# A dense layer between two routed stages: q, x and y reach their transposed form through memory and VectorE instead of TensorE

## The reference, cut to what matters

```python
# q, k, v: (8, 8, 576, 64); x: 4608 tokens x 512; w_in: 512 x 2048; w_out: 2048 x 512
kv = einsum('bhsd,bhse->bhde', k, v)
o = einsum('bhsd,bhde->bhse', q, kv)
o = o / sqrt(mean(o * o, axis=-1) + 1e-6) * g_norm
x = o.transpose(0, 2, 1, 3).reshape(4608, 512)
h = x @ w_in
y = (maximum(h, 0) + alpha * minimum(h, 0)) @ w_out          # dense layer
e = argmax(y @ w_gate); p = softmax(y @ w_gate)[e]; s = sigmoid((y @ w_output_gate)[e])
out = p * s * (maximum(y @ w1[e], 0) @ w2[e])                # routed layer, 8 experts, F = 1024
```

## Time and profile before

| | |
|---|---|
| median of 3 runs | 1503.25 us (1499.38 to 1505.24) |
| the profiled execution's own time | 1500.92 us |
| its span | 1499.1 us |
| granted TensorE clock, mean | 0.994 of full speed |
| TensorE busy with matmuls | 1468.6 us, 98% |
| VectorE, ScalarE, GpSimd busy | 48%, 33%, 9% |
| dense tiles | from 30.3 us to about 966 us |
| a dense tile in the middle (tile 5's start to tile 6's) | 427.1 to 506.5 us |
| DMA | 104.5 MB, 100,516 packets |

### The profile page before, as it was taken

The page is one execution under the profiler, slowest core; times in us unless marked ns, Lnnn a source line. Parts: engine busy times, 40 slices in busy tenths (PEclk is TensorE's granted clock), DMA queues, the critical chain, the costliest instruction groups (busy, mean ns, idle before and its releaser), DMA issues.

```text
span 1499.1 us, 27268 instructions
## 1 busy us (share of the span) xinstructions
PE 1468.6 (98%) x8553; PEld 1277.5 (85%) x8554; DVE 723.5 (48%) x1796; ACT 491.3 (33%) x994; POOL 127.6 (9%) x143
## 2 busy tenths in 40 slices
PE   7899999999999999999999999999999999999997
PEld 6788989888898989898989898887888888888886
DVE  3585555565656465645555655663122114444411
ACT  3442232323232323223222221433233234444422
POOL 1000000000000000000000000112111111111111
PEclk8999999999999999999999999999999999999999
DMA  8532121102121102213100000524123114444410
GB/s 193 136 95 70 33 75 33 43 2 75 33 75 33 43 2 61 46 36 71 31 13 23 1 22 1 146 88 156 44 91 106 43 37 149 155 142 157 152 41 32
DMA packets 100516, 104.51 MB, mean 70 GB/s; under 512 B 55296, under 2 KB 75920, under 8 KB 100434
## 3 DMA queue, kind: packets, MB, share of 16 engines
q1 hardware_dynamic: 91618, 80.99, 19.6%
q0 software_dynamic: 7872, 21.09, 4.4%
q10 hardware_dynamic: 944, 1.33, 0.4%
HBM read 84.04 MB, written 20.65 MB: 70 GB/s over the span
## 4 chain that ended last, share of the span: by engine, by line
PE 90%; DMA 4%; DVE 2%; ACT 1%; issue 1%; SPq 1%; POOL 0%; ACTq 0%; POOLq 0%; DVEq 0%
PE psAcc L1346 25%; PE psH L1334 24%; PE psAcc L1469 15%; PE psH L1448 14%; PE psO L1458 2%; PE psO L1279 2%; PE psO L1249 1%; PE psQ L1429 1%; PE psQ L1265 1%; DMA AR<-rows,uid 1%; PE psY L1297 1%; DMA lists<-meta,slot 1%; PE psY L1289 1%; PE psY L1306 1%; DMA AR<-in_v_dram 1%
## 5 line engine op out<-in xcount | busy, mean ns | idle before, releaser
L1346 PE MATMUL psAcc<-W,XG 128*128 128x512 f32 x1728 | 438.9, 399 | 0.0
L1334 PE MATMUL psH<-XG,W 128*128 128x384 f32 x2304 | 436.3, 337 | 2.2 <-DVE W L958 1.4
L1334 PEld LDWEIGHTS psH<-XG,W 128*128 128x128 f32 x2304 | 408.4, 188 | 18.0 <-issue 2.7
L1346 PEld LDWEIGHTS psAcc<-W,XG 128*128 128x128 f32 x1728 | 313.7, 188 | 66.1 <-issue 6.0
L683 ACT ACTIVATE XG<-AR 128x128 fp32r<-128x128 f32 (+1 forms) x384 | 132.1, 364 | 639.9 <-DVE AR L988 634.2
L985 DVE TENSOR_SCALAR AR<-psH,acol 128x384 f32<-128x384 f32 x192 | 118.4, 617 | 296.0 <-PE psH L1334 296.0
L1448 PE MATMUL psH<-W,XG 128*128 (+1 forms) x996 | 250.4, 400 | 0.0
L1469 PE MATMUL psAcc<-W,XG 128*128 (+1 forms) x984 | 243.4, 396 | 0.0
L1469 PEld LDWEIGHTS psAcc<-W,XG 128*128 128x128 f32 x984 | 182.9, 189 | 37.3
L1448 PEld LDWEIGHTS psH<-W,XG 128*128 128x128 f32 x996 | 180.8, 188 | 36.8 <-DVE W L966 0.4
L1153 DVE TENSOR_TENSOR XG<-psO,XG 128x512 fp32r<-128x512 f32 x82 | 56.6, 690 | 222.1 <-ACT XG L742 218.8
(11 more groups left out here) (200 smaller groups left out, 873.3 us busy)
## 6 DMA issues: line engine op xcount, KB each, us to landing
AR<-in_moe_w_dram SPq DMA_DIRECT2D x68, 512.0 KB, 4.9
AR<-in_k_dram SPq DMA_DIRECT2D x16, 576.0 KB, 5.4
rows<-AR SPq DMA_DIRECT2D x36, 256.0 KB, 2.1
AR<-in_q_dram SPq DMA_DIRECT2D x32, 256.0 KB, 3.1
AR<-in_v_dram SPq DMA_DIRECT2D x14, 576.0 KB, 6.8
AR<-in_moe_w_in_dram SPq DMA_DIRECT2D x16, 256.0 KB, 2.9
AR<-in_moe_w_out_dram SPq DMA_DIRECT2D x16, 256.0 KB, 3.5
AR<-in_v_dram ACTq DMA_DIRECT2D x2, 576.0 KB, 9.3
```

The source lines that it names most:

```text
L1334: mm = pe.matmul(psH[f % 2][:, 0:TILE], w_in_v[:, wp, cc, f * P:(f + 1) * P], xT[:, b, xp, cc, :], start=(cc == 0 and (wp, xp) == PARTS[0] ...
L1346: mm = pe.matmul(psAcc[m][:, :], gT[:, f % 2, gp, m * P:(m + 1) * P], w_out_v[:, wp, f, :], start=(f == 0 and (gp, wp) == PARTS[0]), stop= ...
```

## The change

Tiles 1 to 11 no longer use PE transposes for q, x and y (the first tile's q and x, and the last tile's y, keep theirs). A 32x32 transpose on VectorE turns only squares within a quarter of the partitions, so the data is brought into memory order that makes this enough. q is loaded as blocks: partition quarter `quad` holds model dimensions 128 quad to 128 quad + 127, in runs of 32 floats (128 bytes), by 16 DMAs a tile, or 32 where the tile spans two batches; `q_turn` transposes each group into `qT`. Scaled x goes out to a scratch tensor `xr` in three DMAs and comes back in twelve (`turn_x`, `fetch_x`), `x_turn` writes it to `sq_sb`, and `x_evacuate` and `x_low` are two instructions each because the norm's weight now depends on the parity of the block (`gcol` has two columns). y, already stored to `rows`, comes back in twelve DMAs (`fetch_y`) and `y_turn` fills `yT`. The model dimension is thereby permuted over partitions, so `w_in` (four DMAs in place of one per chunk) and the gate weights (`wgq`) are loaded in the same order. `load_kv`'s first half moves ahead of `load_q`; `normalise`, `scale_rows`, `parts_copy`, `logit_parts` and `logits` move by a step or so; `wide_logits` moves from step 14 of tile 0 to step 0 of tile 1.

The diff, cut to its core:

```diff
+            def load_q(i, c):
+                a = 3 * i + c
+                if a == 1:
+                    sp.wait_ge(q_tr, TG)
+                else:
+                    sp.wait_ge(qT_set, TG * (a - 1))
+                for bl, s0, t0, n in q_place(c):
+                    src = q[2 * i + bl, :, s0:s0 + 32 * n, :].rearrange("(c r) (t i) (k n) -> r k i c t n", r=2, i=32, k=2)
+                    for quad in range(4):
+                        for cc in range(CH):
+                            sp.dma_start(q_blocks[32 * quad:32 * quad + 32, cc, t0:t0 + n, :],
+                                         src[quad // 2, quad % 2, :, cc, :, :]).then_inc(q_blocks_in, 16)
+            def turn_x(a):
+                for j in range(TG):
+                    sp.wait_ge(xn_set, 3 * a + j + 1)
+                    sp.dma_start(xr[j * P:(j + 1) * P, :], o_sb[:, j, :]).then_inc(x_saved, 16)
+            def fetch_x(a):
+                sp.wait_ge(x_saved, 16 * TG * a)
+                for j in range(TG):
+                    for quad in range(4):
+                        sp.dma_start(o_sb[32 * quad:32 * quad + 32, j, :].rearrange("p (t n) -> p t n", t=4),
+                                     by_quadrant(xr[j * P:(j + 1) * P, :])[quad]).then_inc(x_back[j], 16)
+            def fetch_y(t):
+                sp.wait_ge(y_saved, 16 * TG * (t + 1))
+                for m in range(TG):
+                    src = by_quadrant(rows[TILE * t + P * m:TILE * t + P * (m + 1), 0:DM])
+                    for quad in range(4):
+                        sp.dma_start(y_sb[32 * quad:32 * quad + 32, m, :].rearrange("p (t n) -> p t n", t=4),
+                                     src[quad]).then_inc(y_back[m], 16)
...
-                sp.dma_start(st[:, 0:DM].rearrange("p (c n) -> p c n", c=CH),
-                             w_in[:, f * P:(f + 1) * P].rearrange("(c p) n -> p c n", p=P)
-                             ).then_inc(stage_in[f % 2], 16)
+                for quad in range(4):
+                    sp.dma_start(st[32 * quad:32 * quad + 32, 0:DM].rearrange("p (c n) -> p c n", c=CH),
+                                 w_in[P * quad:P * quad + P, f * P:(f + 1) * P].rearrange("(c i) n -> i c n", c=CH)
+                                 ).then_inc(stage_in[f % 2], 16)
...
             for f in range(5, FC):
                 load_dense(f)
+                if f == FC - 2:
+                    turn_x(1)
...
                 if before:
                     store_y(t - 1)
+                    fetch_y(t - 1)
+                else:
+                    fetch_x(1)
+                if kv:
+                    load_kv(4 * i + 2 * c + 2, 2 * i + c + 1, 0)
                 if ahead and (kv or c == 0):
                     load_q(*nxt(*nxt(i, c)))
                 if kv:
-                    for half in range(2):
-                        load_kv(4 * i + 2 * c + 2 + half, 2 * i + c + 1, half)
+                    load_kv(4 * i + 2 * c + 3, 2 * i + c + 1, 1)
+                if before and ahead:
+                    turn_x(t + 1)
+                    fetch_x(t + 1)
...
# ScalarE, x_evacuate: two halves from sq_sb, where one read psY
-                act.wait_ge(x_tr, 3 * a + j + 1)
+                    act.wait_ge(x_turned, 3 * (a - 1) + j + 1)
+                for k in range(2):
+                    ins = nc.scalar.activation(by_parity(xT[:, b, 0, :, j * P:(j + 1) * P])[:, k, :, :], src[:, k, :, :],
+                                               ACT.Copy, scale=gcol[:, k:k + 1])
...
+            def q_turn(i, c, j):
+                a = 3 * i + c
+                dve.wait_ge(q_blocks_in, q_count(i, c))
+                dve.wait_ge(o_mm, 3 * a + j)
+                V.transpose(out=qT.rearrange("p c (t i) -> p c t i", i=32), in_=q_blocks[:, :, 4 * j:4 * j + 4, :]
+                            ).then_inc(qT_set, 1)
+            def x_turn(a, j):
+                dve.wait_ge(x_back[j], 64 * a)
+                dve.wait_ge(x_lo, 3 * a + j)
+                V.transpose(out=sq_sb.rearrange("p (c t i) -> p c t i", c=CH, i=32), in_=turned(o_sb[:, j, :])
+                            ).then_inc(x_turned, 1)
+            def y_turn(t, m):
+                dve.wait_ge(y_back[m], 64 * (t + 1))
+                dve.wait_ge(lg_parts, 3 * t + m)
+                V.transpose(out=yT.rearrange("p c (t i) -> p c t i", i=32), in_=turned(y_sb[:, m, :])).then_inc(yT_set, 1)
...
# VectorE, the order in a tile
                     step(i, c, f)
+                    if ahead and g in (0, 1, 2):
+                        q_turn(*nxt(i, c), g)
                     if ahead and g in (1, 2, 3):
                         squares(a, g - 1)
-                    if before and f in (1, 3, 5):
-                        yT_copy(t - 1, (f - 1) // 2)
-                    if before and f in (2, 4, 6):
-                        parts_copy(t - 1, (f - 2) // 2)
+                    if t == 1 and f == 0:
+                        wide_logits()
+                    if before and f in (4, 5, 6):
+                        parts_copy(t - 1, f - 4)
+                    if before and f in (3, 4, 5):
+                        y_turn(t - 1, f - 3)
...
                     if ahead and f in (13, 14, 15):
+                        x_turn(a, f - 13)
                         x_low(a, (i + c + 1) % 2, f - 13)
...
# TensorE, side(s)
-                    if ahead and g in (0, 1, 2):
-                        q_transpose(ia, ca, g)
-                    if before and s in (1, 3, 5):
-                        y_transpose(t - 1, (s - 1) // 2)
-                    if before and s in (2, 4, 6):
-                        logit_parts(t - 1, (s - 2) // 2)
+                    if before and s in (5, 6, 7):
+                        logits(t - 1, s - 5)
+                    if before and s in (4, 5, 6):
+                        logit_parts(t - 1, s - 4)
-                    if ahead and s >= 13:
-                        x_transpose(a, s - 13)
```

More of the change, by code:

```diff
@@ L205, in attention_dense_moe_routed_moe @@
         xn_set = sem("xn_set")
+        x_saved = sem("x_saved")
+        x_back = [sem(f"x_back{j}") for j in range(TG)]
+        x_turned = sem("x_turned")
         x_tr = sem("x_tr")
@@ L217, in attention_dense_moe_routed_moe @@
         y_saved = sem("y_saved")
+        y_back = [sem(f"y_back{m}") for m in range(TG)]
         y_tr = sem("y_tr")
@@ L329, in load_kv, with load_q_rows @@
                 load_rows(sp, v, b, half, v_rows, kv_in)
-            def load_q(i, c, first=False):
+            def load_q_rows():
                 for j in range(TG):
[L333 to L338, removed]
+                    sp.dma_start(q_sb[:, j, :].rearrange("s (h d) -> s h d", h=H),
+                                 q[0, :, j * P:(j + 1) * P, :].rearrange("h s d -> s h d")).then_inc(q_in[j], 16)
@@ L362, in _ @@
             load_rows(sp, k, 0, 1, k_first, kv_in_1)
-            load_q(0, 0, first=True)
+            load_q_rows()
             load_dense(0)
             load_dense(1)
-            for r in range(2):
-                sp.dma_start(gcol[r * D:(r + 1) * D, :], g_norm.rearrange("(d o) -> d o", o=1)).then_inc(first_in, 16)
-            sp.dma_start(arow[:, :], alpha.rearrange("(f p) -> f p", p=P)).then_inc(first_in, 16)
+            sp.dma_start(arow[FC:FC + 2, :].rearrange("k (r i) -> k r i", r=4),
+                         g_norm.rearrange("(k i) -> k i", k=2).unsqueeze(1).to_broadcast([2, 4, 32])).then_inc(first_in, 16)
+            sp.dma_start(arow[0:FC, :], alpha.rearrange("(f p) -> f p", p=P)).then_inc(first_in, 16)
             load_kv(2, 1, 0)
@@ L875, in yT_copy @@
-            def yT_copy(t, m):
-                dve.wait_ge(y_tr, 3 * t + m + 1)
-                V.tensor_copy(yT, psY[:, :].rearrange("p (c n) -> p c n", c=CH)).then_inc(yT_set, 1)
+                src = by_parity((FIRST_X[j][:, :] if is_first(a) else sq_sb).rearrange("p (c n) -> p c n", c=CH))
+                for k in range(2):
+                    ins = V.scalar_tensor_tensor(out=by_parity(xT[:, b, 1, :, j * P:(j + 1) * P])[:, k, :, :],
+                                                 in0=src[:, k, :, :], scalar=gcol[:, k:k + 1],
+                                                 in1=by_parity(xT[:, b, 0, :, j * P:(j + 1) * P])[:, k, :, :].bitcast(F32),
+                                                 op0=ALU.mult, op1=ALU.subtract)
@@ L1018, in tile @@
                         dense_low(f + 2)
-                    if not before and f == 14:
-                        wide_logits()
                     if ahead and f in (13, 14, 15):
+                        x_turn(a, f - 13)
                         x_low(a, (i + c + 1) % 2, f - 13)
@@ L1270, in q_times_kv @@
                 a = 3 * i + c
-                pe.wait_ge(qT_set, 3 * a + j + 1)
-                if not is_first(a):
+                if is_first(a):
+                    pe.wait_ge(qT_first, j + 1)
+                else:
+                    pe.wait_ge(qT_set, 3 * (a - 1) + j + 1)
                     pe.wait_ge(o_set, 3 * a + j)
```

(3 more changed lines are left out.)

166 lines of the change are left out of this document (82 added, 84 removed).

## The result

The changed kernel took 1506.88 us (median of 20 runs, 1503.42 to 1511.26) against 1503.40 us for the kernel before (20 runs): ratio 1.0022, 95% interval 1.0013 to 1.0032. It is slower by 2 to 5 us; 1499, a small gain, was forecast. 1506.88 lies inside the 1491 to 1508 that the forecast gave its own sum, but on the other side of no change. The span of the profiled execution is 1504.3 us, 5.2 more than before.

What follows compares the result with a forecast made beforehand. TensorE was taken to bound the kernel (98% busy, 90% of the chain). Gains of 13.7 and 1.2 us against 12 lost in tile 0 gave -2.9 us, forecast 1499 us; range 1478 to 1522.

Steps and rivals of the forecast that it cites:

- sum: Whole kernel: -13.7 us in ten middle tiles, -1.2 in tile 11, +12 in tile 0, together -2.9; chance 0.40.
- Start of tile 0: Before tile 0: about 1.3 us late, from some 6 more issues before alpha's load and x's instructions in halves.
- Tile 0's queue: SyncE in tile 0: 32 q issues take 13.5 us, 7.8 more, before dense chunk 5; hidden(6) about 9 us late.
- The end of tile 0: Late tile 0: no room on VectorE for three q_turn and three x chains, +3.5 us, less 0.6 for a q group.
- Start of a middle tile: From hidden(15) through the next tile's early steps: q_times_kv(0) at H + 5.33, 0.25 and 1.21 won, 1.46 us in all.
- H: The start of a `hidden`; for the tile's end and next start, times count from that of step 15.
- End of a middle tile: Steps 13 to 15: x's chain makes VectorE steps 4.53 us, next hidden(0) at H + 7.6; x groups win -0.09 us.
- Middle tiles together: Tiles 1 to 10: each wins 1.46 - 0.09 = 1.37 us, ten of them 13.7 us.
- The transpose's price: VectorE, 512 float32 elements on 128 partitions: 0.68 us, range 0.42 to 1.24; rivals cheap 0.10, dear 0.17.
- Short runs: q's 128-byte DMA runs: 18 ns each, hidden; rival says over 90 ns, k and v late, 1512 us upwards, chance 0.09.
- Tile 11 and the tail: Tile 11 wins 1.2 us from y alone; the tail (routed units) keeps its instructions.
- ideal gain of 42.6 us: Tiles 0 to 11: 99 groups of four TensorE transposes removed at 0.43 us, if TensorE never waits for their replacements.

Runs made afterwards that it cites:

- e2: The changed kernel with x's transpose, high and low parts at steps 10, 12, 14 instead of 13, 14, 15 in tiles 1 to 10; 1490.4 us, ratio 0.9914.
- e8: The changed kernel plus 95 useless TensorE transposes in tile 0 behind output(3), where TensorE idles; 1504.6 us, ratio 1.0025 to the kernel before.
- e9: The changed kernel plus 118 useless TensorE transposes in tile 0, leaving no gap before hidden(5); 1505.7 us, ratio 1.0029 to the kernel before.
- e11: As e5, with tile 0's x chain split so that VectorE does each low part after the next step's work; 1464.8 us, ratio 0.9764.
- e5: The changed kernel with tile 1's q loads on GpSimd, early x chain, and the next tile's first q turn at step 8 (tiles 1 to 9); 1467.7 us, 0.9787.
- e4: The changed kernel with the 32 q loads for tile 1 issued by GpSimd instead of SyncE; 1496.7 us, ratio 0.9953 to the kernel before.
- e10: The changed kernel with q loaded by rows and transposed by TensorE as before, x chain late; 1499.1 us, ratio 0.9981 to the kernel before.
- e6: The changed kernel with q loaded by rows and transposed by TensorE as before, x chain early; 1482.5 us, ratio 0.9873 to the kernel before.

## Why the prediction was wrong

The sum was -2.9 us and the measured difference is +3.5 (5.2 between the two profiled spans, 8.1 above the sum). Of the 8.1, tile 0 and its start give 4.6 (16.6 us lost, 12 forecast), the middle tiles 4.3, and what follows them -0.8. The waits were those named. Two terms failed in size, the queue of tile 0 and the end of a middle tile; with either one right the sum would have been about +1.5 us, near no change. One mechanism was not named, the lower clock behind an idle stretch.

- **Start of tile 0**: 1.3 us late, measured 1.0. This confirms little: e2, e8 and e9, whose code is the same up to there, started tile 0 at 30.4 to 32.4 us.
- **Tile 0's queue, the first step that failed.** `hidden(6)` was to come 9 us late, 1.3 of it from the start; it came 13.0 late beyond the start, 5.3 more than forecast. Four parts make up the difference. q's row in the queue grew from 5.7 to 16.0 us, as its issues were priced at 0.42 us from the earlier trace rows and follow each other every 0.50: 2.5 us. `w_in` by four DMAs a chunk was counted before alpha's load, but not for chunk 4, which stands ahead of q's row: 1.3 us. From the first issue of chunk 5 to ScalarE's start on it 4.8 us passed instead of 5.6: -0.8. And from `hidden(5)` to `hidden(6)` it took 12.4 us instead of 10.1, most of it at the lower clock: 2.2. The forecast had no term for what an idle TensorE does to its clock.
- **The end of tile 0**: +2.9 forecast, +2.7 measured. Right. In e11, where VectorE doesn't wait for ScalarE inside the chain, `hidden(15)` to the next `hidden(0)` is 1.4 us shorter.
- **Start of a middle tile**: 1.46 us forecast, 1.53 on average up to `hidden(13)`. `q_times_kv(0)` at H + 5.38 (5.33), steps 2, 3 and 13 at 5.08, 5.08 and 4.19 us. Right. That the 0.92 us of waiting there was the larger part of what q could give was not seen: e5 took it away and won 1.18 us a tile. (Tile 5 took 79.6 us before, not 79.3, and 78.5 after.)
- **End of a middle tile, the second step that failed**: -0.09 forecast, -0.59 measured on average. Steps 13 and 14 won their 0.86; the next `hidden(0)` came at H + 8.06 or a little later, not 7.6. The transposes (0.68 forecast, 0.70) account for 0.02 us a chain. The halves of x's high and low part were priced at 418 and 413 ns from the 256-element rows; they take 503 and 482. Unlike those rows they carry a column of scales; they also read and write every second block, and no run parts the two. A VectorE step with a chain lasts 4.66 us, not 4.53, and three times 0.13 is most of the 0.46. The forecast had named this as something that would make it wrong. The Trainium skill (ScalarE: Activation LUTs, What ACT_TABLE_LOAD costs) states about 93 ns for each operand of one value per partition; the 84 ns between two rows of the same size here agree with it, and the forecast had no such term.
- **Middle tiles together**: -13.7 forecast, -9.4 measured; the end's term is the difference.
- **The transpose's price** was put between 0.42 and 1.24 us. The upper end, which the Trainium skill's figure (VectorE: DVE Perf Modes, The three transpose paths) gave for bf16 scaled by four, did not hold: 0.70 us for float32, 512 elements. The nearest row of the trace was the better guide.
- **Short runs**: not dear. In 49 to 58 us, with 128-byte loads in flight, the DMA engines were a third busy, and in e4 the same loads on another queue kept no dense chunk back.
- **Tile 11 and the tail**: -1.2 forecast, -2.0 measured. Tile 11 wins 1.2 up to `hidden(13)`, as forecast. The rest is within the scatter: from tile 11's start to the end, the changed kernel and the experiments took 598.9 to 604.8 us.

Most of the ideal gain of 42.6 us was thus lost in three places, each tested: in the queue ahead of dense chunk 5 (e4: 0.7% back), in three chains on consecutive steps of VectorE (e2: 1.1% back), and in one transpose that the next tile's first attention product waits for (e5: 0.6% back). With all three mended the ratio is 0.9787, 32 us of the 42.6. Much of what is missing lies in tile 0, which takes 86.4 us in e5 and 81.4 in the kernel before.

## What to carry to other kernels

Work moved off the bounding engine pays only where its results are early: three chains of 2.5 us on consecutive steps cost TensorE more than they freed, and the same chains with a free step between them cost nothing. A load cut into pieces is paid per piece in the queue that issues it; count every load of the change in that queue, weights too, and look at the stretch where a load is already waited for. Price an instruction from a row with the same kinds of operands and the same access pattern, not only the same size. And work that only fills an engine's wait must end before the wait does.

## What the runs showed of the hardware

- A VectorE transpose of 32x32 squares, 128 x 512 float32, takes 0.70 us, the same within 3 ns for q, x and y: little more than the 0.68 us of an elementwise instruction of that size.
- ScalarE copies of 256 elements with a column of scales took 84 ns more than those without (503 against 419 ns), VectorE's two-input instructions 67 ns more (482 against 415). The rows differ in access pattern too.
- Gaps included, a DMA issue for q (3 dimensions, 128-byte runs) took 0.50 us on SyncE in the row of 32, and 0.57 on GpSimd in e4. SyncE's median without the gap was 0.44 us for q and 0.43 for a piece of `w_in`.
- In e8 the granted clock was still 1.00 for the 2.2 us in which TensorE idled, and 0.50 from shortly after it had begun to work again: what a gap costs can fall on the work behind it.
- The same order of work met different clocks in single executions: between `hidden(0)` and `hidden(6)` of tile 0 the granted clock was 0.50 for 10 us in e10, and never in e6.
